# Expert 0 of a routed feed-forward kernel: w_out's low rows one tile later, weights lowered ahead of x, seven search visits at other places

## The reference

```
f = sigmoid(f_logit); state = f*state + k v^T; y = q state        # gated linear attention, 8 heads of 48
logits = x @ w_gate                                               # 8 experts
# all (token, expert) pairs in order of falling logit: a token takes the expert
# if neither is taken/full; each expert gets exactly cap = 384 tokens
out[mask_e] = relu(x[mask_e] @ w1[e]) @ w2[e]                     # w1: 384x1024, w2: 1024x384
h = out @ w_in; g = where(h>0, h, exp(min(h,0))-1); g @ w_out     # w_in: 384x2048, w_out: 2048x384
```

## Time and profile before

| | us |
|---|---|
| median of 3 runs | 818.69 |
| profiled execution, whole | 818.85 |
| its span (first to last instruction) | 816.9 |
| TensorE busy (PE) | 779.2 (95%) |
| VectorE busy (DVE) | 456.6 (56%) |
| ScalarE busy (ACT) | 465.5 (57%) |
| GpSimd busy (POOL) | 531.1 (65%) |

### The profile page before, as it was taken

The page is one execution under the profiler, slowest core; times in us unless marked ns, Lnnn a source line. Parts: engine busy times, 40 slices in busy tenths (PEclk is TensorE's granted clock), DMA queues, the critical chain, the costliest instruction groups (busy, mean ns, idle before and its releaser), DMA issues.

```text
span 816.9 us, 17723 instructions
## 1 busy us (share of the span) xinstructions
PE 779.2 (95%) x5989; PEld 742.6 (91%) x5989; DVE 456.6 (56%) x1136; ACT 465.5 (57%) x980; POOL 531.1 (65%) x500
## 2 busy tenths in 40 slices
PE   7999996399999999999999999999999999999995
PEld 7888885389999999999999999999999999999995
DVE  6999997784665576358535863675365622330001
ACT  5777766052774287428733773377347635853653
POOL 8888882576875278528852885278538854954652
PEclk9999998599999999999999999999999999999998
DMA  6776692220130041004000400040004004100000
GB/s 197 215 219 209 197 337 99 102 92 2 63 123 1 30 155 30 11 21 164 21 23 7 166 19 30 4 173 10 30 22 153 11 30 154 30 1 31 1 1 29
DMA packets 33739, 65.68 MB, mean 80 GB/s; under 512 B 4560, under 2 KB 20944, under 8 KB 33280
## 3 DMA queue, kind: packets, MB, share of 16 engines
q1 hardware_dynamic: 27072, 50.36, 18.5%
q0 software_dynamic: 3136, 9.64, 3.6%
q10 hardware_dynamic: 3456, 4.72, 1.6%
HBM read 55.26 MB, written 9.44 MB: 79 GB/s over the span
## 4 chain that ended last, share of the span: by engine, by line
PE 85%; DVE 5%; POOL 3%; issue 3%; ACT 1%; SPq 1%; DMA 0%; DVEq 0%; ACTq 0%; POOLq 0%
PE o_ps L1470 8%; PE o_ps L1472 8%; PE o_ps L1471 8%; PE m_ps L1450 6%; PE m_ps L1454 6%; PE m_ps L1458 6%; PE o_ps L1410 3%; PE m_ps L1392 3%; PE o_ps L1412 3%; PE o_ps L1411 3%; PE m_ps L1390 3%; PE m_ps L1393 3%; PE a_ps L640 3%; PE y_ps L607 3%; PE xr_ps L583 2%
## 5 line engine op out<-in xcount | busy, mean ns | idle before, releaser
L1091 POOL TENSOR_TENSOR t_lo<-whole,t_hi 128x384 fp32r<-128x384 f32 x190 | 211.4, 1114 | 86.3 <-ACT t_hi L1176 84.4
L1119 POOL TENSOR_TENSOR whole<-whole,below 128x384 f32<-128x384 f32 x126 | 137.8, 1094 | 131.2 <-ACT below L1195 130.3
L1470 PE MATMUL o_ps<-w_out_hi,t_hi 128*128 128x384 f32 x378 | 127.7, 338 | 0.9 <-POOL t_lo L1091 0.8
L1472 PE MATMUL o_ps<-w_out_hi,t_lo 128*128 128x384 f32 x378 | 126.6, 335 | 0.0
L1471 PE MATMUL o_ps<-w_out_low,t_hi 128*128 128x384 f32 x378 | 126.4, 334 | 0.0
L1450 PE MATMUL m_ps<-y_hi,w_in_hi 128*128 128x384 f32 x288 | 99.6, 346 | 0.0
L1454 PE MATMUL m_ps<-y_hi,w_in_low 128*128 128x384 f32 x288 | 96.6, 335 | 0.0
L1191 ACT ACTIVATE whole<-m_ps 128x384 f32<-128x384 f32 x96 | 47.0, 490 | 64.9 <-PE m_ps L1458 62.3
L1175 ACT ACTIVATE whole<-m_ps 128x384 f32<-128x384 f32 x48 | 23.6, 492 | 94.5 <-PE m_ps L1390 81.0
L1195 ACT ACTIVATE below<-below 128x384 f32<-128x384 f32 x128 | 67.3, 526 | 16.8 <-ACT below L1192 0.8
L1470 PEld LDWEIGHTS o_ps<-w_out_hi,t_hi 128*128 128x128 f32 x378 | 71.0, 188 | 2.2 <-issue 1.7
(11 more groups left out here) (278 smaller groups left out, 1882.7 us busy)
## 6 DMA issues: line engine op xcount, KB each, us to landing
w_raw<-w SPq DMA_DIRECT2D x16, 1536.0 KB, 6.4
f_in<-f_t SPq DMA_DIRECT2D x48, 96.0 KB, 2.3
k_in<-k_t SPq DMA_DIRECT2D x48, 96.0 KB, 2.4
q_in<-q_t SPq DMA_DIRECT2D x48, 96.0 KB, 2.4
v_in<-v_rows SPq DMA_DIRECT2D x24, 192.0 KB, 2.7
x_scratch<-x_row ACTq DMA_DIRECT2D x24, 192.0 KB, 2.6
w_in_raw<-w_in SPq DMA_DIRECT2D x1, 3072.0 KB, 11.5
w_out_raw<-w_out SPq DMA_DIRECT2D x1, 3072.0 KB, 21.0
```

What stands on the lines that cost most here:

```text
L1091: nc.gpsimd.tensor_tensor(t_lo[n % RING][:], whole[n % 3][:], t_hi[n % RING][:], ALU.subtract).then_inc(lo_made, 1)
L1119: nc.gpsimd.tensor_tensor(tile[:], tile[:], below[m % 2][:], ALU.subtract).then_inc(g_made, 1)
L1470: nc.tensor.matmul(o_ps[t][:], hi[:, rows], w_out_hi[:, m, :], start=(m == 0), stop=False)
L1472: ins = nc.tensor.matmul(o_ps[t][:], lo[:, rows], w_out_hi[:, m, :], start=False, stop=(m == MI - 1))
```

## The change

Three things in expert 0. GpSimd lowers no rows of w_out between hidden tiles 0 and 1; the rows come two after each of tiles 1 to 5 and one after tile 6. VectorE starts to lower expert 1's weights when inner tile 10's low part is made instead of 11's, and does all three pieces of w1 and the first of w2 before x's first part, and the other two of w2 before x's second part. Search visits 1 to 7 stand at other places of TensorE's order.

```diff
             elif start:
-                visits = {("h", 3): 0, ("h", 4): 1, ("h", 5): 2, ("y", 2): 3, ("y", 3): 4, ("h", 7): 5, ("y", 5): 6, ("y_end", 0): 7,
+                visits = {("h", 3): 0, ("y", 1): 1, ("y", 2): 2, ("h", 6): 3, ("h", 7): 4, ("y", 4): 5, ("y_end", 0): 6, ("y_end", 2): 7,
                           ("g01", 0): 8, ("g", 2): 9, ("g", 4): 10, ("o", 0): 11, ("g", 6): 12, ("g", 7): 13, ("g", 8): 14, ("g", 9): 15}
...
                 gather_at = 9 if start else 3 if last else 7
+                rows_by = [ROWS_AHEAD, ROWS_AHEAD] + [min(ROWS_AHEAD + 2 * n, MI - 1) for n in range(1, MH - 1)] + [MI - 1]
                 for n in range(MH):
                     lower(k, n)
                     if start:
-                        for row in range(ROWS_AHEAD + 2 * n, min(ROWS_AHEAD + 2 * n + 2, MI - 1)):
+                        for row in range(rows_by[n], rows_by[n + 1]):
                             lower_w_out(row)
...
-                dve.wait_ge(lo_made, k * NT + MH + (12 if start else 6 if last else 10))
+                dve.wait_ge(lo_made, k * NT + MH + (11 if start else 6 if last else 10))
                 if start:
-                    lower_first(k + 1, [0])
+                    lower_first(k + 1)
+                    lower_second(k + 1, 0)
                     x_lower_part(k + 1, 0, r_ps)
-                    lower_first(k + 1, range(1, PIECES))
-                    x_lower_part(k + 1, 1, r_ps)
-                    lower_second(k + 1, 0)
-                    x_lower_part(k + 1, 2, r_ps)
                     lower_second(k + 1, 1)
                     lower_second(k + 1, 2)
+                    x_lower_part(k + 1, 1, r_ps)
+                    x_lower_part(k + 1, 2, r_ps)
                     return
```

## The result

The changed kernel takes 821.38 us (median of 7 runs, 821.10 to 821.57), the kernel before beside it 818.69 us (7 runs, 818.49 to 818.86): a ratio of 1.0032, with an interval of 1.0021 to 1.0044. It is slower by 2.7 us. The prediction said 819.0 and no measurable change; its range ended at 820.1.

The account below looks back on a forecast made before the run. TensorE, busy 95%, was the bound, waiting on GpSimd in hidden tiles and tail. From 818.85: 0 (rows) + 0.26 + 0.11 (visits) - 0.1 (tail) gave 819.12, in median terms 818.96, said as 819.0; range 817.9 to 820.1.

Parts of the forecast that it names:

- The next visits have more room than this: Search visits after visit 8 shift with TensorE and add nothing; visit 9 was answered over 0.5 us early.
- the visits' 0.37 us: Re-placed visits: +0.26 us for visit 6 behind the wait at ("y_end", 0), +0.11 for visit 8 waiting for VectorE.
- The other passing on, from 249.67 to the end: TensorE from ("o", 13) to the last expert: no wait of weight, so every shift is passed on unchanged.
- The rows of w_out: Expert 0's hidden tiles: GpSimd's work is equal, tile 7's low part ends at 197.64 as before; gain 0.
- Rival C: At ("y_end", 0) GpSimd isn't the bound; both waits there and the tail's go: -2.4 us, 816.3; chance 0.07.
- VectorE's tail: Expert 1's weights lowered one tile earlier, ahead of x: 0.1 us gained, between 0.87 gained and 1.6 lost.
- the four pieces ahead of x: VectorE from 238.07: w1's pieces at 1.23, 1.71, 1.71 and w2's first at 1.70 us, ending at 244.4.
- The wait for tile 13: TensorE at ("o", 13), 0.87 us lost; GpSimd's low part was to end at 249.4 instead of 249.52.
- x's second part: VectorE's low part, done at 248.6 for transposes at 248.55: 0.1 to 0.2 us late, hidden.
- Rival B: Tail: low parts of 12 and 13 fall between VectorE's pieces, the 0.87 us wait goes; 818.2; chance 0.20.
- Rival D: Tail: all GpSimd operations from 239.12 take 1.99 us, ("o", 13) starts at 251.25; 820.6; chance 0.07.
- Rival E: TensorE's clock falls for 5 us after the merged wait of 1.4 to 1.7 us; 821.5; chance 0.04.

Follow-up runs that it names:

- after_w2_later: The changed kernel with the load of expert 1's w2 held until inner tile 9's product is made; 819.77 us, ratio 1.0005.
- rows_only: The kernel before with w_out's rows one tile later, visits and VectorE's tail as before; 818.61 us, ratio 1.0001.
- rows_spread: The kernel before with w_out's rows none after tile 0, one after each of tiles 1 to 6, five after tile 7; 817.10 us, ratio 0.9983.
- tail_only: The kernel before with VectorE's earlier start and weights ahead of x alone; 819.01 us, ratio 1.0009.
- before_pad240: The kernel before with 240 semaphore increments more in TensorE's program, 15 behind each visit of the first search; 832.91 us.
- visits_1_5: The kernel before with search visits 1 to 5 alone re-placed, 6 and 7 as before; 819.2 us, ratio 1.0004.
- rows_spread_tail2_w2_later: rows_spread with VectorE's tail one tile earlier, x's first part ahead of w2, and expert 1's w2 load held; 816.51 us, ratio 0.9974.

## Why the prediction was wrong

- The time was outside the range for one step: "The next visits have more room than this (visit 9 was answered over 0.5 us early) and shift with TensorE." From visit 8 at 204 us to the tail at 245 I passed the visits' 0.37 us on through a dense stretch, with no term of its own in the sum, and I had looked there at VectorE's answers alone. The stretch held the fetch of TensorE's own instructions, and the visits made it late: 1.70 us in the profiled run. after_w2_later takes it away; its median, on another chip, is 819.77, 1.6 us under the changed kernel's and inside the range. What makes the fetch late by way of the visits stays open. The other passing on, from 249.67 to the end, held: +2.25 us at expert 1's first product, +2.2 for the span.
- The rows of w_out: right, 0 us (rows_only 1.0001), one wait of 1.49 us for two, the product at 197.6 and not at 196.2. Rival C falls; but rows_spread shows that 1.4 us were there to be had with fewer rows ahead of tile 7, which I had left aside with "the work is equal": equal for this order only.
- The visits: right in size (+0.33 for +0.37, visit 8 about 0.1 us late), wrong in that this was all they did.
- VectorE's tail: the sign failed. I took a gain of 0.1 and it cost 0.45 (tail_only 0.4). The term mis-sized is the four pieces ahead of x: 6.35 us against 7.2. I had read the 5.14 us of the earlier trace rows as three times 1.71 and then walked 1.23, 1.71, 1.71. But that line holds one cheap piece and two dear ones, as the single instructions of the kernel before show:

```profile
315.89 1.22 DVE L1554 TENSOR_TENSOR w_low<-w_raw,w_hi 128x1024 fp32r<-128x1024 f32 x1 [6.36 <-POOL t_lo L1091]
...
317.03 2.04 DVE L1554 TENSOR_TENSOR w_low<-w_raw,w_hi 128x1024 fp32r<-128x1024 f32 x1
...
318.99 2.03 DVE L1554 TENSOR_TENSOR w_low<-w_raw,w_hi 128x1024 fp32r<-128x1024 f32 x1
```

So I counted the cheap one twice. The changed kernel has the same three prices (1.24, 2.04, 2.03), and w2's first took 2.16 for 1.70. And the walk had x's first part at 244.9 with its reader, the transposes at 245.07, 0.17 us behind, a margin that I didn't write down: I compared only the second part with its reader. The wait for tile 13 did shrink (by 0.72 of 0.87), and x's second part was 0.3 us late where I had 0.1 to 0.2, hidden. Rival B falls with this: the tail gained nothing.
- Rival D's crowding was there (four of GpSimd's six operations of the tail took 1.99 to 2.13 us), but not at its place: TensorE lost 0.15 us at tile 13 and 1.1 us at x's second and third part. ("o", 13) started at 251.89, beyond D's mark of 251, by the stop at 230 us; without its 1.70 us it would have been at 250.2. Rival E falls, with a granted clock of 1.00 through the 1.49 us and the 1.87 us. That the time came within 0.12 us of its figure of 821.5 is chance.

## What to carry to other kernels

A dense stretch isn't an empty one: before a small shift is passed on through it, look in the DMA view for the instruction packets, and ask what bulk load stands beside each; this kernel has one every 7 to 30 us from the routing on, and a load of 1.5 MB in front of it cost TensorE 1.7 to 2.0 us. Here it helped to issue the load behind the fetch. When a merged line of the timeline gives a price, look at its single instructions: a mean can hide a cheap one that is already in it. When an order puts several pieces ahead of a short operation, compare every short operation with its own reader, not only the last.

## What the runs showed of the hardware

- The 16,384-byte fetch near 230 us took 0.93 to 1.40 us, and where TensorE stopped it went on 1.3 to 1.5 us after the fetch's end. Its start, for the same place in the program, ranged from 223.66 to 230.29 us (before_pad240, all 14 us later, apart).
- A time can have two values 2.2 us apart with nothing changed but the chip or the run: the kernel before was at 818.3 to 818.9 or at 820.3 to 821.2 us on one chip, and visits_1_5 at 819.1 or 821.2. The profiled late kernels have the stop at 230 us; no run of the kernel before that was late was profiled.
- VectorE and GpSimd side by side in SBUF slow each other. In the changed kernel's tail both work without a pause: VectorE's 128x1024 pieces start 1.95 to 1.97 us apart (from 241.02 on) and GpSimd's 128x384 operations 1.95 to 1.96 (from 241.94 on), where one alone takes 1.23 and 1.01 us. At the edges of such a stretch the price varies: VectorE's 128x1152 took 2.16 us in the changed kernel beside a GpSimd operation of 2.12, and 1.35 us in rows_spread_tail2_w2_later (at 242.44) beside one of 2.19; GpSimd's takes 1.02 by itself. The Trainium skill (GPSIMD Engine Reference, Specifications and Key points) states the sharing without such a price; the trace agrees with it.
